# Attention into two MLPs on one core: norm sum in split float32r, last output tiles stored one by one, first key sums on GpSimd

## Chip, cores and metric

One core of a Trainium2 chip. The metric is the device time of one execution in microseconds; the median of the runs counts.

## The reference

Four batches, eight heads, 576 positions, head dimension 64. Attention has two parts that are added: one over keys, queries and values averaged by fours, repeated back, and one over the nearest positions.

```python
q_d, k_d, v_d = (z.reshape(B, H, S // 4, 4, D).mean(axis=3) for z in (q, k, v))
out = repeat(softmax(q_d @ k_d.T / 8) @ v_d, 4) + softmax(where(|i - j| < 4, q @ k.T / 8, -1e9)) @ v
x = out as (2304, 512)
h = x @ w_in;  g = max(h, 0) + alpha * min(h, 0);  x = g @ moe_w_out              # d_ff 2048
xn = x / sqrt(mean(x * x, axis=-1) + 1e-6) * rms_g
g = xn @ w_gate;  y = (g * sigmoid(g) * (xn @ w_val)) @ moe2_w_out                # d_ff 1536
```

## The kernel before

Every float32 matrix product of the MLPs is made of three float32r products (hi x hi, hi x lo, lo x hi): ScalarE rounds a tile to its high part, VectorE or GpSimd subtracts to get the low part. Weights come in pieces of 128 x 512; `piece_hi` (L647, ScalarE) and `piece_lo` (L840 VectorE, L596 GpSimd) split them.

**The front.** The first group of attention (batch 0, first half of the positions, four pairs of heads p = 0 to 3) has nothing to lie beside. Its order is written out by hand for each engine as FIRST_PE, FIRST_ACT and FIRST_DVE (L80 to L82). A letter is a step, the digit the pair: A turns q and k (three fills on TensorE, L1087; ScalarE copies them out, L682; VectorE sums keys and queries by fours, L889 and L891); B the scores (L1098, L1101) and their maxima (L865 to L874); P and E the exponentials on ScalarE; F the normalising on VectorE (L847 to L854), which multiplies `sm` by the reciprocal sums; C turns the probabilities (L1109, L1113, copied out L696); D the product with v (L1125, L1130), its copy `od` (L701) and the sum into `xbuf` (L927); X the split of `xbuf` into `xhi` (L706) and `xlo` (L934); H and L the high and low part of a weight piece; K the coefficients; W on TensorE are filling matmuls (L1192). GpSimd makes the masks (L586, L592), sums v by fours into `vd` (L616 to L620, three adds with a semaphore between them), and then splits pieces 6, 8, 10 wholly and the low parts of others. TensorE's B needs `kd` and `qd` of its pair; D needs `vd`. The split of the x tiles ends the front: `up(1)` of the first block also needs the low part of piece 2 (the third piece), which VectorE makes as L2.

**The first MLP** runs over eight blocks of 288 tokens. In each, 16 chunks of `up` (L1144) and, two chunks behind, `down` (L1158); beside them the attention steps of the next group, put in slots. ScalarE makes the two ReLUs and `g1hi` (L717, L718, L724), VectorE the leaky sum and `g1lo` (L945, L952). ScalarE also splits two weight pieces a chunk in the first block (L650).

**The second MLP** runs over six blocks of 384 tokens with 12 chunks: `up2` (L1229, 24 matmuls), `silu` (L755), product with the value branch (L986), `g2hi` and `g2lo` (L758, L989), `down2` two chunks behind (L1244, nine matmuls: three tiles of 128 tokens, three products each). The RMS norm of the next block lies inside the block before: NORM1 and NORM2 (L101) name the chunk after which each of its parts is done: first the squares (L736, ScalarE) and their sum over four rows (L965, VectorE), second on TensorE the sum over partitions by a matrix of ones (L1169, float32), third the root (L740) and the reciprocal and scaling (L970, L974). At the end of a block `split_xn` (L749, L980) and `y_out`: ScalarE copies tiles 0 and 2 (L764), VectorE tile 1 (L995), all three after the block's last matmul, and SyncE stores them (L479).

Of the kernel before, what the change touches and what calls it, by code (L numbers as in the profile page):

```python
# [5 lines left out]
def attention_into_two_mlps_kernel(nc: bass.Bass, q, k, v, w_in, w_leaky, alpha, w_gate, w_val, w_out, rms_g, out):  # L6
# [11 lines left out]
    P = 128  # L18
# [62 lines left out]
    FIRST_ACT = "A0 A1 A2 P0 E0 A3 P1 E1 C0 H0 P2 E2 D0 P3 E3 C1 X0 K0 C2 D1 C3 D2 X1 D3 X2 X3 H2 H4"  # L81
    FIRST_DVE = "A0 A1 B0 A2 B1 F0 A3 B2 B3 F1 D0 F2 F3 X0 D1 L0 D2 X1 D3 X2 X3 L2 L4"  # L82
# [18 lines left out]
    NORM1, NORM2 = (5, 10, 10), (6, 7, 7)  # L101
# [7 lines left out]
    with ctx:  # L109
# [10 lines left out]
        ones = sb("ones", [P, P])  # L120
        loaded = ExitStack()
# [54 lines left out]
        ss = sb("ss", [P, TB2], f32, part2)  # L176
        rinv = sb("rinv", [P, TB2], f32, part2)
# [39 lines left out]
        s_kd = sem("s_kd")  # L217
        s_qd = sem("s_qd")
# [28 lines left out]
        s_ss = sem("s_ss")  # L247
        s_ms = sem("s_ms")
# [10 lines left out]
        s_g2_used = sem("s_g2_used")  # L259
        s_y_act = sem("s_y_act")  # L260
# [307 lines left out]
        def _(pool):  # L568
# [52 lines left out]

            mask_half(0)
            for p in range(G):
                v_sums(0, p)
# [15 lines left out]
        def _(act):  # L640
# [96 lines left out]

            def norm_root(i):
                act.wait_ge(s_ms, i + 1)
                act.activation(rinv[:, :], ms_b[:, 0:TB2], ACT.Sqrt, bias=eps6[:, :], scale=1.0 / DM  # L740
                               ).then_inc(s_rms, 1)
# [18 lines left out]
            def y_out(i):  # L760
                act.wait_ge(s_g2_used, C2 * (i + 1) + BEGUN)
                act.wait_ge(s_y_out, 16 * YT * i + BEGUN)
                for t in (0, 2):
                    act.activation(ysb[:, t, :], y_b[t][:, :], ACT.Copy).then_inc(s_y_act, 1)  # L764

            def first_mlp(b, half, group, last=False, pieces=False):
                for c in range(C1):
                    run_steps(group, 2 * c)
                    chunk_relu(b, half, c)
                    run_steps(group, 2 * c + 1)  # L770
                    chunk_hi(b, half, c)
                    if pieces:
                        for n in SPLIT_IN_CHUNK[c]:
                            piece_hi(n)
                    if last:
                        for n in LAST_PIECES[c]:
                            piece_hi(n)
                        if c == NORM1[0]:
                            norm(0)
                        if c == NORM1[2]:  # L780
                            norm_root(0)
                if last:
                    split_xn(0)
                else:
                    split_x(*group)
                acc_out(b, half, last)
# [12 lines left out]
            for kind, p, j in first_order(FIRST_ACT):  # L799
                if kind == "K":  # L800
                    coefficients()
                elif kind == "H":
                    piece_hi(p)
                elif kind == "X":
                    split_pair(0, 0, p)
                elif kind in "PE":
                    first_softmax(kind, p)
                else:
                    attention(0, 0, kind, p, j)
            first_mlp(0, 0, (0, 1), pieces=True)  # L810
# [7 lines left out]
            def second_mlp(i, more):  # L818
                for c in range(C2):
                    chunk2(i, c)  # L820
                    if isinstance(i, int) and i == 0:
                        for n in LAST_PIECES[C1 + c]:
                            piece_hi(n)
                    if more and c == NORM2[0]:
                        norm(i + 1)
                    if more and c == NORM2[2]:
                        norm_root(i + 1)
                if more:
                    split_xn(i + 1)
                y_out(i)  # L830
# [8 lines left out]
        def _(dve):  # L839
# [41 lines left out]
            def attention(b, h, kind, p, j):  # L881
# [4 lines left out]
                if kind == "A" and j == FILLS[h] - 1:  # L886
                    drained(dve, b, h, kind, p, j)
                    if h == 0:
# [74 lines left out]
            def norm(i):  # L963
                dve.wait_ge(s_sq, i + 1)
                dve.tensor_reduce(ss[:, :], sq[:, :].rearrange("p (t s) -> p s t", t=KT), axis=AX.X, op=ALU.add  # L965
                                  ).then_inc(s_ss, 1)

# [24 lines left out]
            def y_out(i):  # L992
                dve.wait_ge(s_g2_used, C2 * (i + 1) + BEGUN)
# [3 lines left out]
            def first_mlp(b, half, group, last=False):  # L997
                for c in range(C1):
# [4 lines left out]
                    if last:  # L1003
# [3 lines left out]
                        if c == NORM1[0]:  # L1007
                            norm(0)
                        if c == NORM1[2]:
                            norm_scale(0)  # L1010
# [29 lines left out]
            def second_mlp(i, more):  # L1040
                for c in range(C2):
# [5 lines left out]
                    if more and c == NORM2[0]:  # L1047
                        norm(i + 1)
                    if more and c == NORM2[2]:
# [12 lines left out]
        def _(pe):  # L1062
# [99 lines left out]
            def norm(i):  # L1162
# [5 lines left out]
                pe.wait_ge(s_ss, i + 1)  # L1168
                pe.matmul(ms_b[:, 0:TB2], ones[:, :], ss[:, :], start=True, stop=True).then_inc(s_ms, 1)  # L1169

            def first_mlp(b, half, group, last=False):
                for c in range(C1):
# [5 lines left out]
                    if last and c == NORM1[1]:  # L1178
# [54 lines left out]
            def down2(i, c):  # L1233
# [7 lines left out]
                for t in range(YT):  # L1241
                    hi, lo = (g[:, c % 3, t * P:(t + 1) * P] for g in (g2hi, g2lo))
                    for j, (g, w) in enumerate(((hi, 0), (hi, 1), (lo, 0))):
                        last = pe.matmul(y_b[t][:, :], g, wpiece(piece, w), start=(c == 0 and j == 0),  # L1244
                                         stop=(c == C2 - 1 and j == 2))
                last.then_inc(s_g2_used, 1)

            def second_mlp(i, more):
                for c in range(C2):
# [3 lines left out]
                    if more and c == NORM2[1]:  # L1253
# [34 lines left out]
```

## Time and profile before

| | us |
|---|---|
| median of 3 runs | 1013.38 (1012.98 to 1015.3) |
| profiled execution, its own time | 1013.07 |
| span of that execution | 1011.3 |
| TensorE busy | 988.5 (98%) |
| VectorE, ScalarE, GpSimd busy | 523.4, 403.4, 113.4 |
| TensorE's share of the chain that ended last | 90% |

The profiled execution is 0.31 us below the median; 1.8 us of its time lie outside the span. TensorE sets the time nearly everywhere. Its busy share is lower in the first three of the 40 slices of the span and in the last one. In the chain VectorE stands with 5%, ScalarE with 2%, and 2% are issue.

### The profile page before, as it was taken

The numbers are of one execution on the slowest core, as the hardware profiler recorded it, in microseconds if no ns is written. First come the engines' busy times: TensorE is split into PE (matmuls) and PEld (weight loads), VectorE is DVE, ScalarE is ACT, GpSimd is POOL, SyncE is SP. The second block draws the span as 40 slices with busy tenths as digits, with TensorE's granted clock in tenths as the row PEclk, the third lists the DMA queues.
The fourth block names the chain that finished last, engine by engine and source line by source line (L and its number), as shares of the span: only waits on it lengthen the run. The fifth ranks groups of instructions, "written<-read, shape, count | busy, mean of one in ns | idle before, by whom it ended". The sixth has DMA issues, their size and how long they took to land.

```text
span 1011.3 us, 19296 instructions
## 1 busy us (share of the span) xinstructions
PE 988.5 (98%) x7207; PEld 939.7 (93%) x7207; DVE 523.4 (52%) x955; ACT 403.4 (40%) x953; POOL 113.4 (11%) x122
## 2 busy tenths in 40 slices
PE   8889999999999999999999999999999999999998
PEld 7789999998999999999999999999999999999997
DVE  6887875765766757666456453242242242242211
ACT  6656444445444445444455443232232232232211
POOL 3665310002200012000011221000000000000000
PEclk9999999999999999999999999999999999999999
DMA  8931311113201032010154400100100100100000
GB/s 165 267 94 37 95 37 36 33 43 82 51 20 48 11 99 59 20 49 2 52 178 149 121 1 24 40 1 23 40 0 24 38 0 27 36 0 29 4 1 31
DMA packets 98800, 52.19 MB, mean 52 GB/s; under 512 B 60564, under 2 KB 92840, under 8 KB 98728
## 3 DMA queue, kind: packets, MB, share of 16 engines
q1 hardware_dynamic: 94584, 50.14, 17.9%
q10 hardware_dynamic: 4144, 1.03, 0.7%
q8 instruction: 51, 0.84, 0.3%
q14 instruction: 21, 0.17, 0.0%
HBM read 41.72 MB, written 9.44 MB: 51 GB/s over the span
## 4 chain that ended last, share of the span: by engine, by line
PE 90%; DVE 5%; issue 2%; ACT 2%; DMA 1%; SPq 0%; ACTq 0%; DVEq 0%
PE banks L1229 30%; PE banks L1158 19%; PE banks L1144 17%; PE banks L1244 15%; PE banks L1098 2%; PE banks L1125 2%; PE banks L1109 2%; PE banks L1087 1%; DVE pos L945 1%; PE banks L1113 1%; PE banks L1130 1%; PE banks L1101 1%; PE banks L1192 1%; DMA q_tok_first<-in_q_dram 1%; DVE sm L901 0%
## 5 line engine op out<-in xcount | busy, mean ns | idle before, releaser
L1229 PE MATMUL banks<-xnhi,W_front 128*128 128x384 f32 x672 | 175.9, 335 | 0.0
L986 DVE TENSOR_TENSOR g<-banks,silu 128x384 f32<-128x384 f32 x72 | 40.1, 557 | 236.6 <-ACT silu L755 236.6
L1158 PE MATMUL banks<-g1hi,W_front 128*128 128x288 f32 x640 | 145.9, 304 | 0.0
L1144 PE MATMUL banks<-xhi,W_front 128*128 128x288 f32 x640 | 144.5, 302 | 1.2 <-DVE W_front L843 1.0
L755 ACT ACTIVATE silu<-banks 128x384 f32<-128x384 f32 x72 | 35.4, 492 | 259.7 <-PE banks L1229 259.7
L1229 PEld LDWEIGHTS banks<-xnhi,W_front 128*128 128x128 f32 x672 | 121.9, 188 | 1.3
L945 DVE SCALAR_TENSOR_TENSOR pos<-neg,coef,pos 128x288 f32<-128x288 f32 x128 | 76.8, 600 | 81.6 <-ACT neg L718 81.5
L1229 PE MATMUL banks<-xnlo,W_front 128*128 128x384 f32 x336 | 112.4, 335 | 0.0
L1158 PEld LDWEIGHTS banks<-g1hi,W_front 128*128 128x128 f32 x640 | 107.7, 189 | 3.6 <-issue 3.6
L1144 PEld LDWEIGHTS banks<-xhi,W_front 128*128 128x128 f32 x640 | 107.5, 189 | 3.1 <-DVE W_front L843 1.3
L717 ACT ACTIVATE pos<-banks 128x288 f32<-128x288 f32 x128 | 52.2, 408 | 130.5 <-PE banks L1144 130.3
L1229 PE MATMUL banks<-xnhi,W_back 128*128 128x384 f32 x384 | 103.2, 339 | 0.0
L1144 PE MATMUL banks<-xlo,W_front 128*128 128x288 f32 x320 | 94.9, 297 | 0.0
L1158 PE MATMUL banks<-g1lo,W_front 128*128 128x288 f32 x320 | 94.9, 297 | 0.0
L724 ACT ACTIVATE g1hi<-pos 128x288 fp32r<-128x288 f32 x128 | 56.5, 441 | 89.1 <-DVE pos L945 88.7
L952 DVE TENSOR_TENSOR g1lo<-pos,g1hi 128x288 fp32r<-128x288 f32 x128 | 59.0, 461 | 53.5 <-ACT g1hi L724 53.5
L1144 PE MATMUL banks<-xhi,W_back 128*128 128x288 f32 x384 | 84.5, 296 | 0.0
L1158 PE MATMUL banks<-g1hi,W_back 128*128 128x288 f32 x384 | 83.8, 301 | 0.8 <-DVE g1lo L952 0.8
L1229 PEld LDWEIGHTS banks<-xnhi,W_back 128*128 128x128 f32 x384 | 69.7, 188 | 1.5
L1244 PE MATMUL banks<-W_front,g2hi 128*128 128x512 f32 x216 | 67.2, 392 | 0.0
L1158 PEld LDWEIGHTS banks<-g1hi,W_back 128*128 128x128 f32 x384 | 63.3, 188 | 2.3 <-issue 1.2
L1144 PEld LDWEIGHTS banks<-xhi,W_back 128*128 128x128 f32 x384 | 64.2, 188 | 0.1
(151 smaller groups left out, 1894.0 us busy)
## 6 DMA issues: line engine op xcount, KB each, us to landing
W_raw<-in_moe_w_out_dram SPq DMA_DIRECT2D x26, 256.0 KB, 4.8
x_scratch<-xbuf SPq DMA_DIRECT2D x8, 576.0 KB, 3.5
xn<-x_scratch SPq DMA_DIRECT2D x6, 768.0 KB, 4.6
out_dram<-ysb SPq DMA_DIRECT2D x18, 256.0 KB, 2.2
vwin<-in_v_dram SPq DMA_DIRECT2D x90, 51.0 KB
W_raw<-in_moe_w_in_dram SPq DMA_DIRECT2D x16, 256.0 KB, 5.6
q_tok<-in_q_dram SPq DMA_DIRECT2D x56, 72.0 KB, 2.1
v<-in_v_dram SPq DMA_DIRECT2D x26, 144.0 KB
```

The source lines that it names most:

```text
L717: act.activation(pos[:, c % 2, :], hb[c % 2][:, 0:TB1], ACT.Relu).then_inc(s_pos, 1)
L724: act.activation(g1hi[:, c % 3, :], pos[:, c % 2, :], ACT.Copy).then_inc(s_ghi, 1)
L755: act.activation(silu[:, c % 2, :], gate_b[c % 2][:, 0:TB2], ACT.Silu).then_inc(s_silu, 1)
L945: dve.scalar_tensor_tensor(out=pos[:, c % 2, :], in0=neg[:, c % 2, :], scalar=coef[:, c:c + 1], in1=pos[:, c % 2, :], op0=ALU.mult, op1=AL ...
L952: dve.tensor_tensor(g1lo[:, c % 3, :], pos[:, c % 2, :], g1hi[:, c % 3, :].bitcast(f32), ALU.subtract).then_inc(s_glo, 1)
L986: dve.tensor_tensor(g2[:, c % 2, :], val_b[c % 2][:, 0:TB2], silu[:, c % 2, :], ALU.mult).then_inc(s_g2, 1)
L1098: pe.matmul(scores[0:QW, e, w * KW:(w + 1) * KW], qT[rows[e], p % 2, q0:q0 + QW], kT[rows[e], p, k0:k0 + KW], start=True, stop=True)
L1109: pe.transpose(turned[0:KW, e, w * QW:(w + 1) * QW], sm[:, e, w * KW:(w + 1) * KW], ident[0:QW, 0:QW])
L1144: last = pe.matmul(hb[c % 2][:, 0:TB1], w, x[:, t, :], start=(t + j == 0), stop=(t == KT - 1 and j == 2))
L1158: last = pe.matmul(acc[t][:, 0:TB1], w, g[:, c % 3, :], start=(c == 0 and j == 0), stop=(c == C1 - 1 and j == 2))
L1229: last = pe.matmul(bank[:, 0:TB2], w, x[:, t, :], start=(t + j == 0), stop=(t == KT - 1 and j == 2))
L1244: last = pe.matmul(y_b[t][:, :], g, wpiece(piece, w), start=(c == 0 and j == 0), stop=(c == C2 - 1 and j == 2))
```

## The change

Norm: a first high part and a low part of the sum of squares are made (ScalarE copy, VectorE subtract) and TensorE multiplies both with a float32r matrix of ones, two matmuls instead of one float32 matmul. The places of the parts move. Output: tiles 0 and 1 have a semaphore of their own. Front: GpSimd makes `kd` of the first group with three adds for each pair (three pairs ahead of the first v sum, the fourth behind it), VectorE only `qd`; H0, H2, L2, F2, D0 and others change places; ScalarE makes the float32r ones between the front and the first block.

```diff
-    FIRST_ACT = "A0 A1 A2 P0 E0 A3 P1 E1 C0 H0 P2 E2 D0 P3 E3 C1 X0 K0 C2 D1 C3 D2 X1 D3 X2 X3 H2 H4"
-    FIRST_DVE = "A0 A1 B0 A2 B1 F0 A3 B2 B3 F1 D0 F2 F3 X0 D1 L0 D2 X1 D3 X2 X3 L2 L4"
+    FIRST_ACT = "A0 A1 A2 P0 E0 A3 P1 E1 C0 P2 E2 D0 P3 E3 C1 H0 X0 K0 C2 H2 D1 C3 X1 D2 D3 X2 X3 H4"
+    FIRST_DVE = "A0 A1 B0 A2 B1 F0 A3 B2 B3 F1 F2 D0 F3 X0 L0 D1 L2 X1 D2 D3 X2 X3 L4"
...
-    NORM1, NORM2 = (5, 10, 10), (6, 7, 7)
+    NORM1, NORM2 = (5, 8, 10), (6, 7, 8)
...
+            def k_sums(p):
+                drained(pool, 0, 0, "A", p, 2)
+                src, dst = kT[:, p, :].rearrange("p (s r) -> p s r", r=FACTOR), kd[:, p, :]
+                pool.tensor_tensor(dst, src[:, :, 0], src[:, :, 1], ALU.add).then_inc(s_kd0, 1)
+                pool.wait_ge(s_kd0, 2 * p + 1)
+                pool.tensor_tensor(dst, dst, src[:, :, 2], ALU.add).then_inc(s_kd0, 1)
+                pool.wait_ge(s_kd0, 2 * p + 2)
+                pool.tensor_tensor(dst, dst, src[:, :, 3], ALU.add).then_inc(s_kd, 1)
+
             mask_half(0)
-            for p in range(G):
+            for p in range(G - 1):
+                k_sums(p)
+            v_sums(0, 0)
+            k_sums(G - 1)
+            for p in range(1, G):
                 v_sums(0, p)
...
+            def norm_hi(i):
+                act.wait_ge(s_ss, i + 1)
+                if not isinstance(i, int) or i > 0:
+                    act.wait_ge(s_ms, i)
+                act.activation(sshi[:, :], ss[:, :], ACT.Copy).then_inc(s_sshi, 1)
...
             def y_out(i):
-                act.wait_ge(s_g2_used, C2 * (i + 1) + BEGUN)
                 act.wait_ge(s_y_out, 16 * YT * i + BEGUN)
                 for t in (0, 2):
+                    if t == YT - 1:
+                        act.wait_ge(s_g2_used, C2 * (i + 1) + BEGUN)
+                    else:
+                        act.wait_ge(s_y_tile, (YT - 1) * i + t + 1)
                     act.activation(ysb[:, t, :], y_b[t][:, :], ACT.Copy).then_inc(s_y_act, 1)
...
+            act.wait_ge(s_consts, 2 + NW)
+            act.activation(ones_r[:, :], ones[:, :], ACT.Copy).then_inc(s_eps, 1)
             first_mlp(0, 0, (0, 1), pieces=True)
...
                 if kind == "A" and j == FILLS[h] - 1:
-                    drained(dve, b, h, kind, p, j)
-                    if h == 0:
+                    drained(dve, b, h, kind, p, 0 if is_first(b, h) else j)
+                    if h == 0 and not is_first(b, h):
                         dve.tensor_reduce(kd[:, p, :], kT[:, p, :].rearrange("p (s r) -> p s r", r=FACTOR),
                                           axis=AX.X, op=ALU.add).then_inc(s_kd, 1)
...
+            def norm_lo(i):
+                dve.wait_ge(s_sshi, i + 1)
+                if not isinstance(i, int) or i > 0:
+                    dve.wait_ge(s_ms, i)
+                dve.tensor_tensor(sslo[:, :], ss[:, :], sshi[:, :].bitcast(f32), ALU.subtract).then_inc(s_sslo, 1)
...
             def y_out(i):
-                dve.wait_ge(s_g2_used, C2 * (i + 1) + BEGUN)
+                dve.wait_ge(s_y_tile, (YT - 1) * i + 2)
...
-                pe.wait_ge(s_ss, i + 1)
-                pe.matmul(ms_b[:, 0:TB2], ones[:, :], ss[:, :], start=True, stop=True).then_inc(s_ms, 1)
+                pe.wait_ge(s_eps, 3)
+                pe.wait_ge(s_sslo, i + 1)
+                pe.matmul(ms_b[:, 0:TB2], ones_r[:, :], sshi[:, :], start=True, stop=False)
+                pe.matmul(ms_b[:, 0:TB2], ones_r[:, :], sslo[:, :], start=False, stop=True).then_inc(s_ms, 1)
...
-                    if last and c == NORM1[1]:
+                    if last and c == NORM1[2]:
                         norm(0)
...
+                    if c == C2 - 1 and t < YT - 1:
+                        last.then_inc(s_y_tile, 1)
...
-                    if more and c == NORM2[1]:
+                    if more and c == NORM2[2]:
                         norm(i + 1)
```

`norm_hi` and `norm_lo` are called after chunk NORM1[1] and NORM2[1], ScalarE's and VectorE's root and scaling after chunk NORM1[2] and NORM2[2] as before; TensorE's sum comes after chunk NORM1[2] and NORM2[2].

## Rows read from the trace of the kernel before

**Rows 1.** Busy time by stretch (stretch, length, engines, granted clock, DMA share, GB/s).

```profile
0.00:34.80 34.80, 26.99 (x306) 24.28 (x307) 23.90 (x48) 23.12 (x93) 18.94 (x40) 1.00 0.86 188
629.00:704.70 75.70, 75.70 (x400) 70.81 (x399) 23.54 (x35) 19.47 (x34) 0.00 (x0) 1.00 0.07 22
```

**Rows 2.** The chain in order of time, second MLP (start us, us, what).

```profile
597.11 2.08 PE banks L1244 x9
599.84 4.17 PE banks L1229 x24
```

**Rows 3.** Waits of TensorE, 34 to 600 us (us in total, times, longest).

```profile
PE banks L1158 <- DVE g1lo L952: 0.8, 1, 0.8
```

**Rows 4.** Timeline of VectorE, a middle block of the second MLP (start us, us, what).

```profile
676.40 2.55 DVE L970 RECIPROCAL rinv<-rinv 128x384 f32<-128x384 f32 x1 [1.33 <-ACT rinv L740]
...
681.12 0.55 DVE L986 TENSOR_TENSOR g<-banks,silu 128x384 f32<-128x384 f32 x1
```

**Rows 5.** Timeline of all engines at the end of the span.

```profile
1006.84 1.09 ACT L764 ACTIVATE ysb<-banks 128x512 f32<-128x512 f32 x2 [4.52 <-PE banks L1244]
1006.84 0.69 DVE L995 COPY ysb<-banks 128x512 f32<-128x512 f32 x1 [3.93 <-PE banks L1244]
1007.47 1.31 SPq L479 DMA_DIRECT2D out_dram<-ysb  x3
```

**Rows 6.** Timeline of GpSimd, front and first block.

```profile
13.10 0.73 POOL L616 TENSOR_TENSOR vd<-v_first 72x256 f32<-72x256 f32 x1 [8.17 <-DMA v_first<-in_v_dram]
13.91 0.72 POOL L618 TENSOR_TENSOR vd<-vd,v_first 72x256 f32<-72x256 f32 x1
...
17.28 1.16 POOL L618 TENSOR_TENSOR vd<-vd,v_first 72x256 f32<-72x256 f32 x1
...
31.79 1.59 POOL L604 TENSOR_TENSOR W_front<-W_raw,W_front 128x512 fp32r<-128x512 f32 x1
...
40.78 1.28 POOL L604 TENSOR_TENSOR W_front<-W_raw,W_front 128x512 fp32r<-128x512 f32 x1 [3.01 <-ACT W_front L650]
```

**Rows 7.** Timeline of VectorE, first half of the front.

```profile
7.81 0.75 DVE L889 TENSOR_REDUCE kd<-kT 128x144 f32<-128x576 f32 x1 [7.81 <-ACT kT L682]
...
14.38 0.46 DVE L865 TENSOR_REDUCE negmax<-banks 96x2 f32<-96x288 f32 x1 [0.57 <-PE banks L1101]
```

**Rows 8.** Timeline of TensorE, front and first block.

```profile
9.46 0.77 PE L1098 MATMUL banks<-kT,qT 64*96 64x102 f32 x12
...
20.18 0.77 PE L1098 MATMUL banks<-kT,qT 64*96 64x102 f32 x12
20.79 0.41 PE L1101 MATMUL banks<-kd,qd 64*96 64x144 f32 x4
...
38.37 0.41 PE L1144 MATMUL banks<-xhi,W_front 128*128 128x288 f32 x1 [1.02 <-DVE W_front L843]
```

**Rows 9.** Timeline of VectorE, second half of the front.

```profile
21.72 0.45 DVE L865 TENSOR_REDUCE negmax<-banks 96x2 f32<-96x288 f32 x1
...
30.09 0.52 DVE L934 TENSOR_TENSOR xlo<-xbuf,xhi 128x288 fp32r<-128x288 f32 x1
...
32.88 0.46 DVE L927 TENSOR_TENSOR xbuf<-banks,od 128x288 f32<-128x288 f32 x1 [0.63 <-ACT od L701]
...
34.02 0.46 DVE L927 TENSOR_TENSOR xbuf<-banks,od 128x288 f32<-128x288 f32 x1 [0.32 <-ACT od L701]
34.40 2.23 DVE L934 TENSOR_TENSOR xlo<-xbuf,xhi 128x288 fp32r<-128x288 f32 x2
36.56 2.36 DVE L843 TENSOR_TENSOR W_front<-W_raw,W_front 128x512 fp32r<-128x512 f32 x2
...
39.20 0.50 DVE L945 SCALAR_TENSOR_TENSOR pos<-neg,coef,pos 128x288 f32<-128x288 f32 x1
```

**Rows 10.** Timeline of TensorE at a long wait in the first block.

```profile
69.26 0.46 PE L1109 MATMUL banks<-ident,sm 96*102 96x96 f32 x3 [1.78 <-DVE sm L905]
```

**Rows 11.** Busy time by stretch, as rows 1, around that wait.

```profile
65.00:74.00 9.00, 7.21 (x49) 6.96 (x48) 7.96 (x13) 5.26 (x11) 5.10 (x5) 0.82 0.01 2
```

More of the change, by code:

```diff
@@ L120, in attention_into_two_mlps_kernel @@
         ones = sb("ones", [P, P])
+        ones_r = sb("ones_r", [P, P], f32r)
         loaded = ExitStack()
@@ L176, in attention_into_two_mlps_kernel @@
         ss = sb("ss", [P, TB2], f32, part2)
+        sshi = sb("sshi", [P, TB2], f32r, part2)
+        sslo = sb("sslo", [P, TB2], f32r, part2)
         rinv = sb("rinv", [P, TB2], f32, part2)
@@ L217, in attention_into_two_mlps_kernel @@
         s_kd = sem("s_kd")
+        s_kd0 = sem("s_kd0")
         s_qd = sem("s_qd")
@@ L247, in attention_into_two_mlps_kernel @@
         s_ss = sem("s_ss")
+        s_sshi = sem("s_sshi")
+        s_sslo = sem("s_sslo")
         s_ms = sem("s_ms")
@@ L259, in attention_into_two_mlps_kernel @@
         s_g2_used = sem("s_g2_used")
+        s_y_tile = sem("s_y_tile")
         s_y_act = sem("s_y_act")
@@ L779, in first_mlp @@
                             norm(0)
+                        if c == NORM1[1]:
+                            norm_hi(0)
                         if c == NORM1[2]:
@@ L825, in second_mlp @@
                         norm(i + 1)
+                    if more and c == NORM2[1]:
+                        norm_hi(i + 1)
                     if more and c == NORM2[2]:
@@ L964, in norm @@
                 dve.wait_ge(s_sq, i + 1)
+                if not isinstance(i, int) or i > 0:
+                    dve.wait_ge(s_sslo, i)
                 dve.tensor_reduce(ss[:, :], sq[:, :].rearrange("p (t s) -> p s t", t=KT), axis=AX.X, op=ALU.add
                                   ).then_inc(s_ss, 1)
+            def norm_lo(i):
+                dve.wait_ge(s_sshi, i + 1)
+                if not isinstance(i, int) or i > 0:
+                    dve.wait_ge(s_ms, i)
+                dve.tensor_tensor(sslo[:, :], ss[:, :], sshi[:, :].bitcast(f32), ALU.subtract).then_inc(s_sslo, 1)
             def norm_scale(i):
@@ L1008, in first_mlp @@
                             norm(0)
+                        if c == NORM1[1]:
+                            norm_lo(0)
                         if c == NORM1[2]:
@@ L1048, in second_mlp @@
                         norm(i + 1)
+                    if more and c == NORM2[1]:
+                        norm_lo(i + 1)
                     if more and c == NORM2[2]:
```

## The prediction

> **What bounds the kernel now.** I read the page first: TensorE is busy for 98% of the span and makes 90% of the chain. Then I cut the span into stretches. In a block of the second MLP TensorE is busy for 75.70 of 75.70 us at the full clock, 2.4 GHz, while VectorE and ScalarE have less than a third each; in the front it is busy for 26.99 of 34.80 us, much of that with filling matmuls, and VectorE and ScalarE have 24 and 23 us [rows 1]. So a saving in the MLPs counts only if it takes work from TensorE's own queue, a saving in the front only if it shortens the chain through VectorE and ScalarE, and at the end only what stands behind the last matmul counts. The chain in order of time shows the first of these places, the timelines of single engines the others.
>
> **The norm sum.** Between two pieces of the chain, 597.11 + 2.08 = 599.19 and 599.84, lie 0.65 us that belong to neither: the float32 matmul of the ones [rows 2]. The row beside it gives 4.17 us for 24 float32r matmuls of the same 384 columns, 0.174 us each [rows 2]. Two of them take 0.35 us, so a norm gets shorter by 0.30 us. There are six. Five lie in blocks of the second MLP where nothing else holds TensorE: 5 x 0.30 = 1.5 us. The sixth lies in the last block of the first MLP. There TensorE waits 0.8 us for g1lo [rows 3], because VectorE does reciprocal and scaling ahead of it; TensorE comes 0.3 us earlier and waits 0.3 us longer. I count it as nothing. If that cover were gone it would be 0.3 us more.
>
> What is added: a copy of 128x384 on ScalarE and a subtraction on VectorE for each norm, about 0.5 us each by the products of the same size [rows 4]. Both stand between chunks where these engines idle for more than half of the time [rows 1], and TensorE asks for the result a chunk (6.25 us) later. Behind the added waits are queued only the next chunk's silu and product. The root and scaling come one chunk later. They hold VectorE from 676.40 to 681.12, 4.72 us [rows 4]; the product of the chunk behind them is then late, but it is wanted only when TensorE refills the same bank, two chunks on, and three `down2` still stand before the next block needs xnlo. Cost nothing; in the first of the six blocks the splits of weight pieces share these chunks, and I allow up to 0.5 us there.
>
> **The last tiles.** After TensorE's last matmul both copies begin at 1006.84; ScalarE needs 1.09 us for two tiles, and SyncE issues three stores from 1007.47 on, in 1.31 us, 0.44 each [rows 5]. With a semaphore for each tile, tiles 0 and 1 are ready six and three matmuls of 2.08/9 = 0.23 us earlier, 1.4 and 0.7 us. Their copies and stores are then past when the last tile's copy, 0.6 us, ends: its store is issued at the place of the first one instead of the third, 2 x 0.44 = 0.87 us earlier. Nothing else is behind it. Bounds 0.5 (the landing, not the issue, decides) and 1.1. In the other blocks TensorE needs those banks only two chunks into the next block: nothing.
>
> **GpSimd's key sums.** No row shows an add of 128x144 with every fourth element. Adds of 72x256 take 0.73 and follow each other after 0.81 us; one of 128x512 takes 1.28 us alone [rows 6]. By the line through the two (0.55 us for 256 elements more) 144 elements take 0.49; the longest two-input row is 1.59 [rows 6]. Bounds 0.45 and 1.6; I take 0.49, since the elements are fewer than in any row. Three with their semaphores, 0.08 each, make 1.7 us: pair 0's `kd`, begun at 7.83 where VectorE began, comes at 9.55 instead of about 8.5 [rows 7]. TensorE's B0 begins at 9.46 [rows 8], behind filling matmuls and the load of pair 1's q, so it moves by 0.1 us. That goes down the chain: A2, P0, B1; VectorE already idles 0.57 us for B1 [rows 7], so the two key sums removed before this point give nothing. The third pair's sums are begun ahead of B1 and end by 14.3, when VectorE has just begun B1's maxima at 14.38 [rows 7] and B2 is still a softmax away; the first v sums, now from 14.3 instead of 13.10 [rows 6] to 16.7, are wanted by D0, which stands behind B3. The fourth pair's sums end at about 18.4, before B3 at 20.18 [rows 8].
>
> **The new order.** From F0 on VectorE is the bound. Without A3's key sum (0.67 effective) B2 is early, but B3 has to await TensorE, which ends B3's matmuls at 21.20 [rows 8]; with the 0.1 us VectorE begins at 21.35 instead of 21.72 [rows 9]: 0.4 us. B3, F1, F2, D0, F3 are the same work in another order, 21.72 to 30.09 [rows 9], a bit less as F1 meets fewer of GpSimd's adds; X0 starts at about 29.6. From there to the first leaky sum of the first block VectorE takes 39.20 - 30.09 = 9.11 us, of which it idles 0.63 and 0.32 [rows 9] and some 0.2 in smaller gaps. L2, one of the two subtractions in the row of 2.36 [rows 9], now stands where it idled: the same work without 1.15 us of gaps, some of which new waits for xhi may keep (0 to 0.5). H2 goes ahead of it on ScalarE; its piece was issued 10 us earlier. So the leaky sum comes 0.5 + 1.15 = 1.65 us earlier, and up to 2.25 where the two subtractions fall outside GpSimd's casts. I take 1.9. TensorE sees it as the wait of 1.02 us for W_front at 38.37 going away and `xlo` coming earlier [rows 8, 9]. The float32r ones cost ScalarE 0.2 us between H4 and the first chunk, where it would wait for TensorE anyway; they wait for GpSimd's masks, done by about 31.5. Next late are the normalised `sm` of the first block, VectorE's work, which moves along: the gain stays.
>
> **Sum.** 1.5 + 0.9 + 1.9 = 4.3 us. The profiled execution's 1013.07 would be 1008.8; it lies 0.31 below the median, so against the median of 1013.38 the forecast is **1009.1**. A measurement of this kernel can tell about 0.2%, 2.0 us, from no change: faster means below 1011.35.
>
> **Rivals.** (1) Strided sums are dear. If an add of 144 strided elements takes what 256 contiguous ones take, 0.73 [rows 6], pair 0's sums need 2.43 us, B0 moves by 0.85 instead of 0.1, and all behind it: 1009.1 + 0.75 = 1009.9. For it: the elements are read 16 bytes apart, which no row shows. The Trainium skill ("GPSIMD Engine Reference", performance pitfalls for Q7 kernels) states that reads with a step of over 8 bytes cost half as much again per element; that alone would make it an estimate of 0.64 an add and 1009.6. No run here shows it so far. Chance 0.2.
>
> (2) The clock. In the first block TensorE waits 1.78 us at 69.26 [rows 10], and in the stretch around it the mean granted clock is 0.82 [rows 11]: for 0.18 x 9 x 2 = 3.2 us it ran at 1.2 GHz, which costs some 1.6 us. The other stretches, shown by 1.00 in the front and in the second MLP [rows 1], had no such fall. With everything two microseconds earlier the fall may not come: 1009.1 - 1.6 = 1007.5. Against it: the wait is made by VectorE and stays. Chance 0.2; that a second one comes, 1010.7, 0.06.
>
> (3) The front's gain doesn't arrive: ScalarE, which now has H0 and H2 amid C and X, holds up `xhi`, or the first block's slots keep their old pace through GpSimd's low parts (L604). Then 1.5 + 0.9 alone: 1011.0. For it: ScalarE has 23.12 of 34.80 us in the front [rows 1]. Against it: that leaves a third of the time, and the new places of H0 and H2 are in its gaps before C2 and D1. Chance 0.12.
>
> (4) Slower. The fourth pair's key sums stand on GpSimd behind nine adds and three v adds: kd3 comes at 7.83 + 12(t + 0.08) + 2.4, t the time of one add. B3 then drives all of VectorE's rest, 16.4 us to the leaky sum. The front's gain is lost when B3 begins after 22.8, and the whole gain when it begins after 25.2: t = 1.17, as in the row of 1.16 that met VectorE's traffic [rows 6]. At t = 1.6, the upper bound, B3 begins at 30.4: 46.8 instead of 39.2, 7.6 less 2.4, 1018.6. Against it: most adds of that kind take 0.73. Chance 0.03.
>
> **Numbers.** Forecast 0.39, rivals 0.2, 0.26, 0.12, 0.03. The range reaches from 1006.8 (the clock's fall gone and the front at 2.25 with a little more) to 1011.4 (rival 3 with 0.4 us for the added work). Faster by over 0.2%: nearly all of the first three and most of the third rival, 0.87; within 0.2%: 0.1; slower: 0.03.
>
> **What the profile of after would show.** Right: TensorE's gap at the norm 0.35 instead of 0.65 us; the third store issued within 0.7 us of the last matmul's end; no wait of TensorE for W_front at `up(1)`; the first leaky sum at about 37.3; key sums of under 0.6 us. Wrong: B0 after 9.8, B3 waiting for `kd`, a wait of `xlo` for `xhi` of over 0.5 us in the front, any wait of TensorE on L1229 or L1244 from the norm moved by a chunk, or a granted clock below 0.99 in another stretch than before.

## The result and the profile after

The changed kernel takes 1011.70 us in the median of 20 runs (1010.29 to 1013.01), the kernel before, measured beside it, 1013.98 us (1012.26 to 1016.06, 20 runs). The ratio is 0.9974 with a 95% interval of 0.9965 to 0.9983: faster by 2.6 us. A ratio compares runs of the same state of the chip, so it can differ a little from the quotient of two medians. The kernel before came out 0.6 us higher here than the 1013.38 from which the forecast counts, so 1011.70 itself stands 0.3 us above the range's upper end of 1011.4. Put on the forecast's footing by the ratio, 0.9974 x 1013.38, the time is 1010.7: inside the range, 0.6 us below 1011.35, under which a time was to count as faster, and 1.6 us above the forecast of 1009.1. The profiled execution took 1012.13 us, with a span of 1010.3.

Where did the 2.6 us come from, and what of the 4.3 didn't come? The chain in order of time, in the second MLP:

```profile
598.79 2.08 PE banks L1296 x9
600.87 4.18 PE banks L1281 x24
605.05 2.08 PE banks L1296 x9
607.13 0.17 PE banks L1220
607.31 0.18 PE banks L1221
607.48 2.62 PE banks L1281 x15
```

Two float32r matmuls of 0.17 and 0.18 us stand now where the float32 one left a gap of 0.65 [rows 2], and a chunk later, as the norm is. From the first matmul of the second MLP to the end of the last one TensorE takes 452.1 us instead of 453.5: 1.4 us.

The timeline of all engines at the end of the span (start us, us, what):

```profile
1005.82 0.60 ACT L795 ACTIVATE ysb<-banks 128x512 f32<-128x512 f32 x1 [3.22 <-PE banks L1296]
...
1006.44 0.69 DVE L1041 COPY ysb<-banks 128x512 f32<-128x512 f32 x1 [3.25 <-PE banks L1296]
1006.44 1.63 SPq L488 DMA_DIRECT2D out_dram<-ysb  x3
...
1006.69 0.39 PE L1296 MATMUL banks<-Wtail,g2lo 128*128 128x512 f32 x1
1007.12 0.60 ACT L795 ACTIVATE ysb<-banks 128x512 f32<-128x512 f32 x1 [0.70 <-PE banks L1296]
```

The first two tiles are copied beside the last matmuls, and the three issues end at 1008.07, 0.99 us after the last matmul's end at 1007.08. Before, they ended at 1008.78, 1.97 us after it [rows 5]. With a landing that is about 0.3 us shorter, the span ends 3.2 us after the last matmul instead of 4.5. So the two parts of the MLP bring 1.4 + 1.3 = 2.7 us, all that was measured, and nothing is left for the front.

In the front, GpSimd's timeline shows the key sums cheap alone:

```profile
7.79 0.45 POOL L634 TENSOR_TENSOR kd<-kT 128x144 f32<-128x144 f32 x1 [2.86 <-ACT kT L704]
8.31 0.56 POOL L636 TENSOR_TENSOR kd<-kd,kT 128x144 f32<-128x144 f32 x1
8.95 0.56 POOL L638 TENSOR_TENSOR kd<-kd,kT 128x144 f32<-128x144 f32 x1
...
17.95 0.99 POOL L638 TENSOR_TENSOR kd<-kd,kT 128x144 f32<-128x144 f32 x1
...
31.97 2.56 POOL L613 TENSOR_TENSOR W_front<-W_raw,W_front 128x512 fp32r<-128x512 f32 x1
```

Three take 1.72 us, from 7.79 to 9.51. But the last two rows ran beside VectorE's work, and took 0.99 instead of 0.56 and 2.56 instead of some 1.3. VectorE's own timeline has the other side of it:

```profile
14.64 0.45 DVE L902 TENSOR_REDUCE negmax<-banks 96x2 f32<-96x288 f32 x1 [1.29 <-PE banks L1151]
...
16.68 0.58 DVE L884 TENSOR_SCALAR sums<-sums 96x8 f32<-96x8 f32 x1
...
20.79 0.69 DVE L909 TENSOR_SCALAR negmaxd<-negmax 96x2 f32<-96x2 f32 x1
...
24.38 0.15 DVE L884 TENSOR_SCALAR sums<-sums 96x8 f32<-96x8 f32 x1
...
24.80 1.21 DVE L888 TENSOR_TENSOR sm_first<-sm_first,rsum 96x612 f32<-96x612 f32 x1
25.93 0.97 DVE L891 TENSOR_TENSOR sm_first<-sm_first,rsum 96x288 f32<-96x288 f32 x1
...
30.96 0.45 DVE L972 TENSOR_TENSOR xlo<-xbuf,xhi 128x288 fp32r<-128x288 f32 x1
...
39.75 0.50 DVE L983 SCALAR_TENSOR_TENSOR pos<-neg,coef,pos 128x288 f32<-128x288 f32 x1
```

A scaling of 96x8 takes 0.15 us alone and 0.58 beside GpSimd. I took for each kind of operation in this stretch its shortest row as its length alone, and summed what the rows have above it. From B1's maxima to the first leaky sum this excess is 5.46 us before and 7.16 us after: 1.70 more. Against it stand the key sum taken away (0.67) and 0.72 less idling inside the stretch. So the stretch is 25.11 us long instead of 24.82 [rows 7, 9], and the leaky sum comes at 39.75 instead of 39.20. Of these 0.55 us, 0.26 stand before B1's maxima already.

TensorE's wait for the weights at `up(1)` is gone, but the one ahead of `up(0)` has grown. Its timeline:

```profile
35.67 0.44 PE L1137 MATMUL banks<-ident,q_tok 96*128 96x96 f32 x3 [1.34 <-DVE xbuf L965]
```

Before, this wait was 0.92 us and ended at 34.58. It awaits D3's sum into `xbuf`, which now stands behind L2; of the kernels below, those with the old orders (norm_only, tail_only, pool_only) have 0.92 too, and front_only has 1.34. With B1 late as well, `up(0)` begins at 35.89 instead of 34.80, and of the 1.02 us saved at `up(1)` 0.07 are left: the next score matmuls begin at 40.09 instead of 40.16.

After that the timelines of TensorE, here its waits in the first block, show two falls of the clock where before had one:

```profile
55.97 0.46 PE L1159 MATMUL banks<-ident,sm 96*102 96x96 f32 x3 [1.72 <-DVE sm L943]
...
69.90 0.46 PE L1159 MATMUL banks<-ident,sm 96*102 96x96 f32 x3 [0.36 <-DVE sm L943]
...
83.73 0.46 PE L1159 MATMUL banks<-ident,sm 96*102 96x96 f32 x3 [1.78 <-DVE sm L943]
```

```profile
54.00:62.00 8.00, 6.28 (x41) 6.03 (x41) 6.18 (x11) 5.68 (x12) 5.06 (x4) 0.79 0.43 114
82.00:90.00 8.00, 6.27 (x48) 6.11 (x50) 5.48 (x9) 5.88 (x13) 5.30 (x4) 0.79 0.00 0
65.00:74.00 9.00, 8.64 (x78) 8.11 (x77) 8.35 (x14) 5.34 (x12) 5.40 (x4) 1.00 0.03 7
```

Those are busy times by stretch, as [rows 1]; the number just ahead of the DMA share, 0.79, is the mean granted clock. In 8 us that is 3.4 us at 1.2 GHz instead of 2.4 GHz, 1.7 us of work not done, each behind a wait of over 1.7 us. The stretch of [rows 11] is free of it now. In this one execution the second MLP starts 1.68 us later than before, though TensorE was 0.07 us early at 40 us: the first `sm` for which it waits comes 0.53 us later (55.97 instead of 55.44), as the leaky sum did, and the second fall does the rest.

### The profile page after: what moved, and what is told of

The parts are those of the page before. It is cut to its first block, busy times and chain, and to the rows that moved or that the text cites. A ratio compares the mean times of both kernels' runs of the same rounds, so it can differ in the third digit from the quotient of the medians.

```text
span 1010.3 us, 19341 instructions
## 1 busy us (share of the span) xinstructions
PE 988.3 (98%) x7207; PEld 941.2 (93%) x7207; DVE 525.5 (52%) x957; ACT 407.0 (40%) x960; POOL 119.6 (12%) x134
## 4 chain that ended last, share of the span: by engine, by line
PE 89%; DVE 6%; issue 2%; ACT 2%; DMA 1%; SPq 0%; DVEq 0%; ACTq 0%
PE banks L1281 30%; PE banks L1208 18%; PE banks L1194 17%; PE banks L1296 15%; PE banks L1148 2%; PE banks L1175 2%; PE banks L1159 2%; DVE pos L983 1%; PE banks L1137 1%; PE banks L1163 1%; PE banks L1180 1%; PE banks L1151 1%; PE banks L1244 1%; DMA q_tok_first<-in_q_dram 1%; ACT W_front L672 0%
```

## The experiments

All times are in us. "The changed kernel" is the one of the diff above; the short diffs are against it unless another is named.

**mlp_parts.** Norm and last tiles as changed, the front as before (`FIRST_ACT` and `FIRST_DVE` too).

```diff
-            for p in range(G - 1):
-                k_sums(p)
-            v_sums(0, 0)
-            k_sums(G - 1)
-            for p in range(1, G):
+            for p in range(G):
                 v_sums(0, p)
```

> Norm by split sums and the last tiles one by one, front as in the kernel before. Theory 1 (the front gives nothing; norm and end are the whole gain): 2.3 to 2.8 us under before, ratio 0.9974, second MLP 1.4 us shorter, end 1.3 us shorter. Theory 2 (the front gives about 2 us, but the profiled run of after hid it behind one more fall of the clock): the ratio is the same 0.9974, but the full change would then be about 4 us under before; it tells the theories apart only together with the next kernel.

Measured: 1010.83 (13 runs), ratio 0.9973 [0.9962, 0.9984], the changed kernel's 0.9974. The two parts bring all of it.

**front_only.** The front as changed, norm and last tiles as before.

```diff
-    NORM1, NORM2 = (5, 8, 10), (6, 7, 8)
+    NORM1, NORM2 = (5, 10, 10), (6, 7, 7)
...
-                pe.matmul(ms_b[:, 0:TB2], ones_r[:, :], sshi[:, :], start=True, stop=False)
-                pe.matmul(ms_b[:, 0:TB2], ones_r[:, :], sslo[:, :], start=False, stop=True).then_inc(s_ms, 1)
+                pe.matmul(ms_b[:, 0:TB2], ones[:, :], ss[:, :], start=True, stop=True).then_inc(s_ms, 1)
```

> Only the front of the change: key sums on GpSimd and the new orders; norm and end as before. Theory 1: within 0.7 us of before, ratio 0.9993 to 1.0005; the first leaky sum of the first block at about 39.7, up(1) right behind up(0) and up(2) at about 41.0. Theory 2: 1.5 to 2 us under before, ratio 0.998.

Measured: 1013.05, ratio 1.0003 [0.9993, 1.0012]. The forecast 1.9 us (0.9981) is excluded.

**order_only** (the front's new orders, all key sums on VectorE; norm and last tiles as before) and **pool_only** (key sums on GpSimd, old orders) split the front.

```diff
-    FIRST_DVE = "A0 A1 B0 A2 B1 F0 A3 B2 B3 F1 F2 D0 F3 X0 L0 D1 L2 X1 D2 D3 X2 X3 L4"
+    FIRST_DVE = "A0 A1 B0 A2 B1 F0 A3 B2 B3 F1 D0 F2 F3 X0 D1 L0 D2 X1 D3 X2 X3 L2 L4"
```

> The new orders alone, all key sums on VectorE as before. Theory 1a (GpSimd's adds stand in the way of VectorE's small and two-input instructions, which takes back what the orders give): without them VectorE reaches the first leaky sum at 38.2 to 38.9, before was 39.20, so 0.3 to 1.0 us under before. Theory 1b (the order itself loses: C1 waits for F1, D0 comes late, X waits): 39.7 or later, as in the change.

> Key sums on GpSimd, the old orders. Theory 1a: the first leaky sum at 39.5 to 40.5, the waits of VectorE's small instructions (L884, L909) of 0.6 to 0.8 us are there as in the change; 0.3 to 1 us over before. Theory 1b: the saved key sum of the fourth pair shows, first leaky sum at 38.5 to 39.0, 0.3 to 0.7 us under before.

Measured: order_only 1.0003 [0.9991, 1.0016], pool_only 0.9996 [0.9986, 1.0007]; neither can be told from no change. The stretch from B1's maxima to the leaky sum is 25.80 in order_only, with an excess of 6.39. Its last row in VectorE's timeline:

```profile
40.54 0.52 DVE L970 SCALAR_TENSOR_TENSOR pos<-neg,coef,pos 128x288 f32<-128x288 f32 x1 [1.06 <-ACT neg L736]
```

L2 closes the gaps between the X steps, but 1.06 us of the stretch are this wait for ScalarE, which was itself waiting for TensorE: from 36 to 42 us the granted clock was 0.50. So the 40.54 is not the sign of theory 1b; VectorE's own part is 24.74. In pool_only the stretch is 24.59, excess 6.32. Two other kernels with the old front give 25.27 and 25.56 (norm_only, tail_only below), so the 24.82 of the profile before was a short one, and some 0.4 us scatters from run to run.

Split at X0, the excess shows what each half of the front's change costs VectorE (to about 0.1 us; the kernels with the old front are the one before, norm_only and tail_only):

| | B1's maxima to X0 | X0 to the leaky sum |
|---|---|---|
| old front | 2.3, 2.8, 2.8 | 3.1, 3.0, 3.1 |
| order_only | 2.7 | 3.7 |
| pool_only | 3.4 | 3.0 |
| changed, front_only | 3.6, 3.4 | 3.6, 3.6 |

The key sums on GpSimd cost VectorE 0.6 to 0.9 us ahead of X0 (more against the profile before, the short one), about the 0.67 that they take off it. The new orders cost 0.5 to 0.7 behind it, about the idling that they fill.

**norm_only** and **tail_only.** One part of the MLP each, all else as before; tail_only keeps this and the copies that belong to it:

```diff
                     if c == C2 - 1 and t < YT - 1:
                         last.then_inc(s_y_tile, 1)
```

> Of the whole change only the norm by split sums with its moved places. By the profile of the changed kernel: the gap of each of five norms 0.34 instead of 0.65 us, the sixth swallowed by the wait for g1lo (0.9 instead of 0.8): 1.4 to 1.5 us under before, ratio 0.9985. Rival (the later root and scaling cost what the matmul saves): second MLP as long as before, 453.5 us, ratio 1.000.

> Only the last three MLP tiles are changed (drained one by one, with the drain and the store of a tile released by that tile's last matmul); the norm and the front stay as before. Theory (the end earns what the profile of after shows, 0.98 us less from the last matmul to the last issue and 0.3 us less landing): about 0.9 to 1.3 us under the kernel before, ratio near 0.9989, and the span ends some 3.2 us after the last matmul instead of 4.5. Rival (the parts overlap: the gain at the end is partly the later start of the drains in the changed kernel, and alone it is worth only the smaller store, 0.3 us): ratio 0.9996 or nearer to one, and an end of 4 us or more. Added to the run with the norm alone (0.9989) the first gives 0.9978 for both, which is to stand against 0.9973 measured for both together.

Measured: norm_only 1011.78, 0.9989 [0.9976, 1.0001]: 1.1 us. tail_only 1012.32 (12 runs), 0.9986 [0.9970, 1.0001]: 1.4 us. Alone, neither interval leaves out 1; their sum, 2.5 us, is the 2.7 us of both together. The end of tail_only, all engines:

```profile
1007.15 0.69 DVE L1029 COPY ysb<-banks 128x512 f32<-128x512 f32 x1 [3.25 <-PE banks L1278]
1007.15 1.63 SPq L488 DMA_DIRECT2D out_dram<-ysb  x3
...
1007.40 0.39 PE L1278 MATMUL banks<-Wtail,g2lo 128*128 128x512 f32 x1
1007.83 0.60 ACT L791 ACTIVATE ysb<-banks 128x512 f32<-128x512 f32 x1 [0.70 <-PE banks L1278]
```

It ends 3.2 us after the last matmul, as the changed kernel does: the gain at the end doesn't need the norm.

**no_v_sums.** GpSimd's value sums of three pairs of the first group are replaced by zeros, to take its two-input adds out of the front.

```diff
+                if is_first(b, 0) and p > 0:
+                    pool.memset(dst, 0.0).then_inc(s_vd0, 1)
...
+                    return
```

> The changed kernel without the three adds of v for pairs 1 to 3 of the first group (GpSimd fills them with zeros, which reads nothing). Contention theory: VectorE's F1 and F2 lose some 1.5 to 2.5 us, F2 ends by 27.3 instead of 29.09, and X0 starts at 29 or before; the first leaky sum gains less, since X and L meet GpSimd's pieces. Rival (F is long by itself or waits for ScalarE): F1 and F2 keep their length.

Measured: 1009.48 (7 runs), 0.9959 [0.9943, 0.9974]. Its F1 in VectorE's timeline, which answers to 24.80 and 25.93 above:

```profile
24.96 0.79 DVE L895 TENSOR_TENSOR sm_first<-sm_first,rsum 96x612 f32<-96x612 f32 x1
25.67 0.45 DVE L898 TENSOR_TENSOR sm_first<-sm_first,rsum 96x288 f32<-96x288 f32 x1
```

B1's maxima to X0 take 14.50 instead of 16.32, with an excess of 1.69 instead of 3.58. That difference, 1.89, is the whole of the 1.82 us by which the stretch is shorter. About 1.5 us arrive in the time (0.9959 against 0.9974, measured in another set of runs; the intervals overlap). Behind X0 its leaky sum waits 0.86 us for ScalarE, in another fall of the clock, so that part can't be compared. So it is GpSimd's adds that hold VectorE up, and not the number of VectorE's own operations. These adds of v are in the kernel before too: the run shows what nine such adds cost, and the table above what the added key sums do.

**quiet_new, quiet_old, keys3_quiet.** GpSimd begins its low parts of the weights only when VectorE is past L4. The front is the changed one, the one before, and the one before with only pair 3's keys on GpSimd; norm and last tiles are as changed in all three.

```diff
-    LO_POOL = list(EARLY_POOL) + [n for n in HI_ORDER if n not in LO_DVE]
+    LO_POOL = [6, 8, 1, 10, 3] + [n for n in HI_ORDER if n not in LO_DVE and n not in (1, 3)]
...
+            pool.wait_ge(s_wlo[0], 3)
             for n in LO_POOL:
```

> The changed kernel, but GpSimd begins its weight pieces (6, 8, then 1, 10, 3) only when VectorE has made L4. Contention theory (GpSimd's two-input and copy instructions hold VectorE's up; X and L took 3.4 us longer in the changed kernel than alone): VectorE's splits of x at 0.45 and of weights at 0.67 to 0.7 each, the first leaky sum at 37 to 38 instead of 39.75, and 1.5 to 2.5 us under the changed kernel, ratio 0.995 to 0.996 to before. Rival (the front's end is set by ScalarE and TensorE, or the late pieces hold up the first block): leaky sum after 39, or a wait of TensorE for GpSimd's low parts in the first block; ratio 0.997 or above.

> Norm and end of the change, the front's orders and key sums of the kernel before, GpSimd's pieces behind L4. Contention theory: X and L lose their 3 us of excess here too; first leaky sum at 36.5 to 37.5, ratio 0.995 to 0.996. If the new orders are worth what their gaps say once contention is gone, it comes 1 us behind quiet_new; if not, both are level.

> As quiet_old, but the key sums of the fourth pair alone are on GpSimd; those of pairs 0 to 2, for which VectorE has idle time, stay on VectorE. Contention theory: TensorE's B0 comes at 9.5 as before, F0 loses 0.3 us to the adds, the saved 0.67 us show: B2 0.3 to 0.4 us earlier than in quiet_old, ratio equal or 0.0003 lower. Rival: GpSimd's three adds cost VectorE as much as they save, equal within 0.1 us at the first leaky sum, counted from B1's maxima.

Measured: 0.9992 [0.9976, 1.0008], 0.9978 [0.9967, 0.9988] and 0.9986 [0.9972, 1.0000], none better than the changed kernel; the 0.995 to 0.996 expected for the first two was missed. The leaky sum comes at 38.62, 38.54 and 37.55, and counted from B1's maxima keys3_quiet reaches it 0.63 us sooner than quiet_old (23.24 instead of 23.87). In the front the edit does what it should. VectorE's and TensorE's timelines of keys3_quiet:

```profile
34.43 1.05 DVE L972 TENSOR_TENSOR xlo<-xbuf,xhi 128x288 fp32r<-128x288 f32 x2
35.55 1.30 DVE L880 TENSOR_TENSOR W_front<-W_raw,W_front 128x512 fp32r<-128x512 f32 x2
...
37.55 0.52 DVE L983 SCALAR_TENSOR_TENSOR pos<-neg,coef,pos 128x288 f32<-128x288 f32 x1 [0.34 <-ACT neg L740]
```

```profile
42.72 0.40 PE L1208 MATMUL banks<-g1hi,W_front 128*128 128x288 f32 x1 [1.69 <-POOL W_front L613]
47.13 0.40 PE L1208 MATMUL banks<-g1hi,W_front 128*128 128x288 f32 x1 [0.67 <-POOL W_front L613]
```

The pairs of subtractions take 1.05 and 1.30 us where they took 2.23 and 2.36 [rows 9], and the leaky sum comes at 37.55, 1.65 us earlier than before. Then TensorE waits 2.4 us for the low parts that were put off.

**cand_old, cand_new.** keys3_quiet with the pieces in the order in which they are wanted, with the old and with the new orders of the front.

```diff
-    LO_POOL = [6, 8, 1, 10, 3] + [n for n in HI_ORDER if n not in LO_DVE and n not in (1, 3)]
+    LO_POOL = [6, 1, 8, 3, 10] + [n for n in HI_ORDER if n not in LO_DVE and n not in (1, 3)]
```

> keys3_quiet with GpSimd's pieces in the order 6, 1, 8, 3, 10 instead of 6, 8, 1, 10, 3. Contention theory: the waits of TensorE for GpSimd's low parts (1.7 and 0.7 us in keys3_quiet) shrink to under 0.5 in all, the first leaky sum stays at 23.2 us behind B1's maxima; 1 to 2 us under the changed kernel, ratio 0.9955 to 0.997. Rival: the front's gain is taken by VectorE's waits for the same work later in the first block, C steps wait longer; ratio 0.9975, as the norm and the end alone give.

> As cand_old, but with the change's new orders. If their filled gap is worth anything once GpSimd is out of the way, the first leaky sum comes 0.3 to 0.8 us earlier behind B1's maxima than in cand_old and the ratio is 0.0003 to 0.0008 lower. Rival: ScalarE and TensorE (D3, up(0)) set the first leaky sum, both level.

Measured: 1010.95 (8 runs), 0.9984 [0.9966, 1.0003], and 1011.34, 0.9992 [0.9977, 1.0008]. The waits for the low parts are gone, and still no gain can be told. cand_new's profile says nothing of the orders: the clock fell in its front, and its leaky sum waited 2.52 us for ScalarE.

These ratios follow the means more nearly than the medians, and runs with a long fall of the clock pull them up. A mean clock of 0.995 or less, with 1013.97 to 1018.38 us, have three of the 12 runs of keys3_quiet, three of the eight of cand_old and four of the 12 of cand_new. Without such runs, on both sides, the means lie 2.0, 2.9 and 2.5 us below the kernel before, that of mlp_parts 2.3 below, and front_only 0.2 above. A few tenths for cand_old are thus not excluded by its five runs; 1.9 us for the front on top of mlp_parts' 2.3 are in none of them.

VectorE's groups from the first leaky sum to the next pair's softmax show why; first before (39.2 to 55.4), then cand_old (37.6 to 55.5):

```profile
L945 DVE SCALAR_TENSOR_TENSOR pos<-neg,coef,pos 128x288 f32<-128x288 f32 x5 | 3.2, 635 | 0.9 <-ACT neg L718 0.9
L952 DVE TENSOR_TENSOR g1lo<-pos,g1hi 128x288 fp32r<-128x288 f32 x4 | 1.8, 455 | 1.5 <-ACT g1hi L724 1.5
...
L912 DVE TENSOR_TENSOR sm<-sm,negmax 96x612 f32<-96x612 f32 x1 | 0.9, 866 | 0.0
```

```profile
L983 DVE SCALAR_TENSOR_TENSOR pos<-neg,coef,pos 128x288 f32<-128x288 f32 x5 | 4.0, 806 | 0.8 <-ACT neg L740 0.8
L990 DVE TENSOR_TENSOR g1lo<-pos,g1hi 128x288 fp32r<-128x288 f32 x4 | 2.8, 702 | 1.5 <-ACT g1hi L746 1.5
L950 DVE TENSOR_TENSOR sm<-sm,negmax 96x612 f32<-96x612 f32 x1 | 1.6, 1584 | 0.0
```

The same ten operations take 5.9 us before and 8.4 in cand_old: GpSimd's low parts meet VectorE there instead of in the front. The leaky sum began at 37.68, 1.52 us earlier than before, but the `sm` for which TensorE waits next releases it at 55.50, against 55.44. In this profile the whole gain is handed back.

What a fall of the clock costs can be read from TensorE's timelines too. Before, with one fall after the wait of [rows 10]:

```profile
55.44 0.46 PE L1109 MATMUL banks<-ident,sm 96*102 96x96 f32 x3 [1.45 <-DVE sm L905]
...
83.21 0.46 PE L1109 MATMUL banks<-ident,sm 96*102 96x96 f32 x3 [0.37 <-DVE sm L905]
...
110.75 0.77 PE L1098 MATMUL banks<-kT,qT 64*96 64x102 f32 x12 [0.57 <-DVE qd L891]
```

and pool_only, with a clock of 1.00 throughout:

```profile
56.15 0.46 PE L1144 MATMUL banks<-ident,sm 96*102 96x96 f32 x3 [1.42 <-DVE sm L934]
...
69.98 0.46 PE L1144 MATMUL banks<-ident,sm 96*102 96x96 f32 x3 [1.80 <-DVE sm L934]
...
83.82 0.46 PE L1144 MATMUL banks<-ident,sm 96*102 96x96 f32 x3 [1.80 <-DVE sm L934]
...
111.36 0.77 PE L1133 MATMUL banks<-kT,qT 64*96 64x102 f32 x12 [0.57 <-DVE qd L920]
```

From the first to the last of these rows it is 55.31 us with the fall and 55.21 without: the slow stretch makes TensorE 1.4 us later at the next `sm`, and it waits 0.37 instead of 1.80 there. VectorE sets the pace, and the fall is nearly free. In the changed kernel's profile the same way takes 56.88 (55.97 to 112.85): its second fall, at 84, has no such wait behind it.

The profiled runs of mlp_parts (span 1013.4, clock 0.991), cand_old (1013.5, 0.993) and cand_new (1016.6, 0.988) had longer falls than their medians can have had. In mlp_parts one stands right in the front:

```profile
34.00:44.00 10.00, 9.07 (x73) 8.72 (x72) 4.57 (x10) 4.71 (x12) 3.42 (x3) 0.55 0.88 246
```

With 9.07 of 10 us busy at little over half the clock, TensorE and not VectorE (4.57) is the bound there, and the fall is paid in full. In six of the 14 profiles a fall lies at the front's end, somewhere from 28 to 44 us. That is why I compare medians and ratios of the parts, and of profiles only what VectorE does of itself there, with its waits for ScalarE named.

## Why the prediction was right, and where it was not

**Direction and range: right**, the range by the ratio, and for the reason given for two of the three parts. The third brought nothing, so rival 3 came true: 1.5 + 0.9 = 2.4 us without the front, 1011.0, against 2.6 us measured. It had a chance of 0.12, which was too little.

**The norm, 1.5 us: right.** Measured 1.4 by the two profiles and 1.1 (norm_only). The gap is 0.35 instead of 0.65, with no wait at the matmuls from the norm a chunk later. The sixth norm gave nothing, as forecast: the wait for `g1lo` behind it is 0.9 instead of 0.8 [rows 3].

**The last tiles, 0.9 us: mechanism right, a bit small.** The issues end 0.98 us earlier, counted from the last matmul, of which 0.87 had been worked out. What the sum left out is the landing of the last store, about 0.3 us shorter. Together 1.3, and 1.4 by tail_only; the upper bound was 1.1.

**The key sums on GpSimd: right in price, too small in effect.** Forecast 1.7 us for three, measured 1.72, with 0.44 us for the add whose two inputs are both strided and 0.56 for the in-place ones. Rival 1 (0.73 an add) is refuted. The Trainium skill ("GPSIMD Engine Reference", performance pitfalls for Q7 kernels) states half as much again per element for such steps, by which my estimate was 0.64; the trace doesn't agree: the three adds take 0.52 on average, near the 0.49 estimated without that surcharge, and the one with two strided inputs is the shortest. TensorE's B0 moved by 0.27 (9.46 to 9.73), of which the forecast had 0.1. The profile names `kT` for its wait of 0.42 us, but B also awaits `kd`, and in all five kernels where GpSimd makes pair 0's `kd` B0 begins 0.21 to 0.24 us after the third add ends, behind a wait of 0.42 to 0.79. Where VectorE makes it, the wait is 0 to 0.28. B0 scatters from run to run, 9.73 to 10.45 with GpSimd and 9.40 to 10.12 with VectorE; the averages are 10.20 and 9.69, so the price at B0 is nearer to 0.5 us than to 0.1. Rival 4 (slower) is refuted: the fourth pair's sums end at 18.94, before B3 at 20.64.

**The front's order, 1.9 us: wrong.** The step that failed is "B3, F1, F2, D0, F3 are the same work in another order ... a bit less as F1 meets fewer of GpSimd's adds; X0 starts at about 29.6". X0 started at 30.96. F1 met no fewer of them: it took 1.21 and 0.97 us, and 0.79 and 0.45 in the one trace from which I had worked. But that trace was a lucky one. VectorE's timeline of norm_only, with the old front:

```profile
25.18 1.13 DVE L881 TENSOR_TENSOR sm_first<-sm_first,rsum 96x612 f32<-96x612 f32 x1
26.24 0.97 DVE L884 TENSOR_TENSOR sm_first<-sm_first,rsum 96x288 f32<-96x288 f32 x1
```

F1 meets the v adds of pair 3, and these begin when that v has been loaded (at 25.23 before and 24.64 in the changed kernel, both after a wait for the DMA), so the key sums ahead of them don't shift them. What the key sums and the v adds that they did shift met is VectorE's small scalings: 0.58 us at 16.68, 0.69 at 20.79, 0.43 at 23.34, against 0.16, 0.17 and 0.39 before. I had costed GpSimd's new work by when its results were due, and not by what VectorE does at that moment. Against the forecast, 0.16 us is missing before B1, 1.20 from B1 to X0 and 1.09 from X0 to the leaky sum (8.79 us instead of 7.70). In that last stretch the forecast took the gaps away without asking what would fill them: idling fell by 0.72 as L2 moved in, and the excess rose by 0.43. pool_only and order_only show the two causes one by one (the table above), and no_v_sums that it is GpSimd's adds: without nine of them the first of the two stretches is 1.82 us shorter. The leaky sum 0.55 us later than before is itself no loss: the old front has it at 39.20, 40.02 and 40.30, the new one at 39.75 and 39.86.

**"The gain stays": wrong too.** Had the front come out as forecast, most of it would have been given back. keys3_quiet and cand_old come near the forecast place of the leaky sum (37.55 and 37.68, forecast 37.3) and bring nothing that can be told from mlp_parts; in cand_old the whole gain is gone by 55 us, because GpSimd's low parts of the weights then lie on VectorE's work in the first block. In these runs the place where the two meet only moved.

Of rival 3's two causes, ScalarE holding `xhi` is visible as one wait of 0.23 us, and only GpSimd is left; but not through the slots' pace, which was the cause named, and through VectorE's operations being held instead.

**The clock (rival 2): open in size.** I had expected the one fall of 1.6 us to stay, to go or to be doubled, and the profiled execution shows it doubled. But the profiles of twelve other kernels show none to several, and a fall ahead of a wait for VectorE cost 0.1 us instead of 1.6. A granted clock below 0.99 in another stretch than before was one of the signs of being wrong that I had named; it came, at 54 to 62 and 82 to 90 us, and the leaky sum at 37.3 did not. How often the falls come in the runs without a profile isn't known in detail; the mean clocks of the changed kernel's runs lie between 0.996 and 1.0, and its fastest run (1010.29) has 1.0 while another with 1.0 took 1012.07.

The rule behind the failed step is in the Trainium skill ("SBUF — State Buffer", who interferes with whom): VectorE in a two-port mode and GpSimd lock each other out of shared ports, whoever issues first holding them for its whole instruction, and VectorE with two inputs from SBUF collides with a GpSimd instruction that reads SBUF. With one SBUF input at most, and outside those modes, VectorE doesn't collide. The trace agrees: 0.15 became 0.58 for a scaling of 96x8 in SBUF and 0.79 became 1.21 for a product of two SBUF tiles, while operations that read the banks kept their 0.45 and 0.78 and the reduction of `sm` in SBUF at 21.39 its 0.78, beside an add. By that rule, each of GpSimd's added two-input adds has a price on VectorE unless VectorE does something of the harmless kind meanwhile. Nothing in the forecast charged it.

Apart from no_v_sums, which leaves out sums that the result needs, no version that was tried beats the changed kernel; mlp_parts (0.9973) is its equal with less in it, and the front's part of the change could be left out.

## What to carry to other kernels

Work moved from VectorE to GpSimd isn't free for VectorE: lay the two timelines side by side and ask, for each of GpSimd's two-input adds, what VectorE runs at that moment. In these traces it cost nothing beside operations that read PSUM, beside reductions, and where VectorE idled. Take savings from the engine that is busy throughout (a float32 matmul made two float32r ones) and from the tail behind its last instruction first; those two arrived in full. And before a gain early in a kernel is counted, find the next wait for the same engine and check that the gain reaches it.

## What was not expected of the hardware

- A strided add of 128x144 with both inputs 16 bytes apart takes 0.44 us on GpSimd, less than an in-place one with a single strided input (0.56). Filling a 72x256 tile takes 0.31. In no_v_sums it left a product of VectorE's alone (0.45 us at 25.67), but not the scaling of 96x8 at 26.04, which took 0.37 instead of 0.15.
- The smallest of VectorE's operations suffer most in proportion: 96x8 and 96x2 scalings went from 0.15 and 0.17 us to as much as 0.83 and 0.69 beside GpSimd's adds.
- The same wait of about 1.8 us is followed by a fall of the clock to 1.2 GHz in one profiled run (before, at 69.26) and not in another (pool_only, at 69.98 and 83.82).
